# Attention inside a fused attention and two-layer kernel on one Trainium2 core: values as stationary operand on four quarters of the array, weights normalised before the turn, a first stage in three sets of banks and six buffers

## The reference, cut to what matters

```python
# batch 4, heads 8, sequence 768, head_dim 64, 8 memory keys; chunks of 32 queries
for c in range(24):
    q_c    = q[:, :, 32*c : 32*c+32]
    k_full = concat(mem_k, k[:, :, max(0, 32*c-16) : min(768, 32*c+40)])   # up to 64 keys
    v_full = concat(mem_v, v[the same rows])
    scores = q_c @ k_full.T / 8
    a = exp(scores - max(scores));  a = a / (sum(a) + 1e-9)
    out[chunk c] = a @ v_full
x = out as 3072 tokens x 512
x = (sigmoid(x @ w_gate) * (x @ w_val)) @ w_out          # d_ff 1536
h = x @ w_in                                             # d_ff 2048
return (P(h) / (Q(h) + 1e-6)) @ w_out2                   # P cubic, Q quadratic
```

## Time and profile before

| | |
|---|---|
| time before, median of 3 | 1200.07 us (1199.81 to 1202.33) |
| the profiled execution, its own time | 1198.92 us |
| its span, first to last instruction | 1196.6 us, mean granted clock 0.998 |
| PE busy | 1168.5 us, 98% |
| PEld, DVE, ACT, POOL busy | 957.1, 904.0, 751.8, 120.7 us |
| stage 0's units, up to the first product of the first chain | 0 to 61.89 us |
| the two stretches of units between chains | 207.48 to 269.89 and 419.70 to 482.19 us |

### The profile page before, as it was taken

How to read it: one execution, slowest core, us unless ns; L and a number is a source line. 1 busy time by engine, 2 the same in 40 slices (tenths; PEclk the granted TensorE clock), 3 DMA queues, 4 the chain that set the end, 5 groups by cost and what they waited for, 6 DMA issues and landing times.

```text
span 1196.6 us, 21070 instructions
## 1 busy us (share of the span) xinstructions
PE 1168.5 (98%) x8160; PEld 957.1 (80%) x8160; DVE 904.0 (76%) x1387; ACT 751.8 (63%) x1224; POOL 120.7 (10%) x150
## 2 busy tenths in 40 slices
PE   8899999899999998999999999999999999999998
PEld 7778888677888866788887888888888888888887
DVE  3686566567666655776558899998998998988987
ACT  2465555455555544555556787877877877877875
POOL 2122322002322200232300000000000000000000
PEclk9999999999999999999999999999999999999999
DMA  8411411742241174332208300200200200200000
GB/s 281 156 53 65 156 54 53 259 144 79 98 168 53 54 256 137 106 132 81 88 18 290 132 1 1 71 1 1 71 0 0 70 0 0 70 0 0 36 1 35
DMA packets 40720, 97.79 MB, mean 82 GB/s; under 512 B 4288, under 2 KB 4288, under 8 KB 40640
## 3 DMA queue, kind: packets, MB, share of 16 engines
q1 hardware_dynamic: 40640, 96.68, 23.6%
HBM read 84.09 MB, written 12.58 MB: 81 GB/s over the span
## 4 chain that ended last, share of the span: by engine, by line
PE 57%; DVE 1%; DMA 1%; SPq 0%; issue 0%; ACT 0%; ACTq 0%
PE ps_h L1263 7%; PE ps_h L1258 7%; PE ps_h L1259 7%; PE ps_y L1302 7%; PE ps_y L1298 7%; PE ps_y L1296 7%; PE ps_h L1152 3%; PE ps_h L1159 3%; PE ps_h L1154 3%; PE ps_y L1197 1%; PE ps_y L1202 1%; PE ps_y L1198 1%; DMA oraw<-wo_l 1%; PE ps_y L1188 0%; PE ps_y L1292 0%; PE ps_y L1290 0%
## 5 line engine op out<-in xcount | busy, mean ns | idle before, releaser
L1152 PE MATMUL ps_h<-xop,wop 128*128 128x512 f32 x504 | 197.2, 391 | 2.9 <-DVE x_raw L809 2.6
L1154 PE MATMUL ps_h<-xop,wop 128*128 128x512 f32 x504 | 196.2, 389 | 0.0
L1159 PE MATMUL ps_h<-xop,wop 128*128 128x512 f32 x504 | 155.9, 390 | 0.0
L1258 PE MATMUL ps_h<-x_split,weights 128*128 128x512 f32 x384 | 149.4, 389 | 0.0
L1259 PE MATMUL ps_h<-x_split,weights 128*128 128x512 f32 x384 | 149.4, 389 | 0.0
L1296 PE MATMUL ps_y<-weights,hid 128*128 128x512 f32 x360 | 140.0, 389 | 0.0
L1298 PE MATMUL ps_y<-weights,hid 128*128 128x512 f32 x360 | 140.0, 389 | 0.0
L788 DVE TENSOR_TENSOR wop<-rawp,wop 128x448 fp32r<-128x448 f32 x144 | 90.9, 660 | 56.6 <-ACT wop L441 56.5
L809 DVE TENSOR_TENSOR x_raw<-ps_h,probs_t 128x512 f32<-128x512 f32 x72 | 49.5, 688 | 87.0 <-PE ps_h L1159 86.6
L675 ACT ACTIVATE tmp<-ps_h 128x512 f32<-128x512 f32 x96 | 57.2, 595 | 92.4 <-PE ps_h L1263 92.4
L1152 PEld LDWEIGHTS ps_h<-xop,wop 128*128 128x128 f32 x504 | 94.6, 188 | 25.3 <-DVE x_raw L809 4.3
(11 more groups left out here) (89 smaller groups left out, 2254.4 us busy)
## 6 DMA issues: line engine op xcount, KB each, us to landing
rawp<-wgv_l SPq DMA_DIRECT2D x36, 512.0 KB, 3.5
oraw<-wo_l SPq DMA_DIRECT2D x72, 256.0 KB, 3.7
unit<-v_l SPq DMA_DIRECT2D x24, 520.0 KB, 5.8
unit<-k_l SPq DMA_DIRECT2D x24, 512.0 KB, 5.7
unit<-q_l SPq DMA_DIRECT2D x24, 256.0 KB, 4.4
x_stage<-y_dram SPq DMA_DIRECT2D x6, 1024.0 KB, 6.0
out<-stage SPq DMA_DIRECT2D x24, 256.0 KB, 2.2
braw<-wb_l SPq DMA_DIRECT2D x11, 512.0 KB, 5.5
```

The source lines that it names most:

```text
L1152: nc.tensor.matmul(dst, w_h[k], xop[:, m, 0, k, :], start=first and k == 0, stop=False, skip_group_check=True)
L1154: nc.tensor.matmul(dst, w_l[k], xop[:, m, 0, k, :], start=False, stop=False, skip_group_check=True)
L1159: last = nc.tensor.matmul(dst, w_h[k], xop[:, m, 1, k, :], start=False, stop=k == 1, skip_group_check=True)
L1258: nc.tensor.matmul(dst, lhs(c, 0), x_split[:, 0, c, :], start=(c == 0), stop=False)
```

## The change

What it does, on each engine:

- The weights are normalised on DVE right after the exponential (a row sum by `tensor_reduce` takes the place of the column of ones, then + 1e-9, reciprocal, multiply), in the units at the sequence's ends after a `memset` of the keys that do not exist. Then they are turned once.
- `weigh_values` has the values stationary (64 x 64) and the turned weights moving (32 columns); row group and bank alternate with the chunk, so that four 64 x 64 quarters are used. Its output is already turned: `stage_x` reads it, and the second `turn` is gone. The scores' products alternate the two banks with the chunk too. The host orders chunks and keys to suit and leaves the column of ones out (512 instead of 520 KB of values to a unit).
- Stage 0: three sets of banks (the third in `ps_y`), six load buffers, loads queued in one go (q and k of unit 6 wait for scores 0, v of unit 6 for the values' products of unit 0), loop written out without fills; warm-up products: 9 ahead, none later. The first chain stands directly behind the last unit's values.
- Stages 1 and 2: still two sets and two buffers; new order of units and thirds, all 36 thirds inside the stretch (4 behind the last values); the splits of `w_out` and the loads are placed anew; the load of the sigmoid table moves from `last_operands` to behind `split_x(T4, 1)` in the first `quad_a` of a stage; in the very first one two pieces of value weights are split there as well.

```diff
+SETS, BUFFERS = 3, 6
+        ps_att = [ps_h[:, 0:2, 0:256], ps_h[:, 2:4, 0:256], ps_y[:, 0:2, 0:256]]
+        def set_of(g):
+            return (g + 1) % SETS if g < UNITS else g % 2
 SP:
+            load_qk(0)
+            load_qk(1)
+            load_v(0)
+            for g in range(2, UNITS):
                 load_qk(g)
+                load_v(g - 1)
+                if g == 4:
+                    load_raw(0)
+            load_v(UNITS - 1)
+            load_raw(1)
 ACT, stage 0:
+            for g in range(UNITS):
+                if g >= 2:
+                    stage_x(g - 2)
+                if g >= 1:
+                    copy_turned(g - 1)
+                exp_scores(g)
+                if g >= 4:
+                    split_w(0, g - 4)
+                if g == 6:
+                    split_x(0, B11)
+            stage_x(UNITS - 2)
+            copy_turned(UNITS - 1)
+            split_x(0, B21)
+            split_x(0, T2, 0)
+            split_x(0, T1, 0)
+            split_x(0, B22, 0)
+            stage_x(UNITS - 1)
 DVE:
             def normalize(g):
+                b, tile = set_of(g), g // B
+                pr = probs[b].rearrange("p h s k -> p s h k")
+                dve.wait_ge(exped, g + 1)
+                if tile == 0:
+                    nc.vector.memset(probs[b][0:CHUNK, :, :, NMEM:NMEM + LEFT], 0.0)...
+                elif tile == NT - 1:
+                    nc.vector.memset(probs[b][P - CHUNK:P, :, :, KEYS - RIGHT:KEYS], 0.0)...
+                nc.vector.tensor_reduce(row[b], pr, AX.X, ALU.add)...
+                nc.vector.tensor_scalar(row[b], row[b], 1e-9, None, ALU.add)...
                 nc.vector.reciprocal(row[b], row[b])...
+                nc.vector.tensor_tensor(pr, pr, row[b] (broadcast), ALU.mult).then_inc(norm_done, 1)
 DVE, stage 0:
+            for g in range(UNITS):
+                if g:
+                    normalize(g - 1)
+                softmax(g)
+                if g >= 5:
+                    split_w(0, g - 5)
+            split_x(0, B11)
+            normalize(UNITS - 1)
+            split_w(0, 3)
+            split_x(0, B21)
+            token_sum(0, T1, 0)
+            token_sum(0, T2, 0)
 DVE and ACT, last_operands(0): split_w(1, 0) and split_w(1, 1) inside; quad_a(0): split_w(1, 2), split_w(1, 3)
 PE:
             def weigh_values(g):
                 for h in range(HP):
                     for c in range(CT):
                         for e in range(2):
+                            rows = slice(KEYS * ((e + c) % 2), KEYS * ((e + c) % 2 + 1))
+                            cols = slice(D * h + CHUNK * (c // 2), D * h + CHUNK * (c // 2 + 1))
+                            last = nc.tensor.matmul(ps_att[b][D * e:D * (e + 1), c % 2, cols],
+                                                    v_sb[at][rows, c, h, :],
+                                                    probs_t[b][rows, h, CHUNK * c:CHUNK * (c + 1)], ...)
 PE, stage 0:
-            warm_up(2 * WARM)
-            attention(0, lambda: warm_up(WARM))
-            warm_up(4 * WARM)
+            warm_up(3 * WARM)
+            for g in range(UNITS):
+                scores(g)
+                if g >= 2:
+                    weigh_values(g - 2)
+                if g >= 1:
+                    turn(g - 1)
+            weigh_values(UNITS - 2)
+            turn(UNITS - 1)
+            weigh_values(UNITS - 1)
+            chain(0, -1)
 PE, stages 1 and 2, for each pair a, b:
                     scores(a)
+                    if p:
+                        turn(b - 2)
+                    fill()
+                    fill()
                     if p:
+                        weigh_values(b - 2)
                     fill()
+                    fill()
                     scores(b)
+                    turn(a)
                     fill()
                     fill()
                     weigh_values(a)
                     fill()
+                    if p < UNITS // 2 - 1:
+                        fill()
+                turn(first + UNITS - 1)
+                fill()
+                weigh_values(first + UNITS - 1)
+                for _ in range(4):
+                    fill()
...
```

More of the change, by code:

```diff
@@ L319, in _ @@
                 n, g = piece_of(s, 0, TA - 2), UNITS * (s + 1)
+                load_oraw(n + 4)
                 load_qk(g + 2)
-                for ahead in (4, 5, 6):
-                    load_oraw(n + ahead)
+                load_oraw(n + 5)
+                load_oraw(n + 6)
                 load_qk(g + 3)
@@ L401, in exp_scores @@
             def exp_scores(g):
-                b = g % 2
+                b = set_of(g)
                 act.wait_ge(shifted, g + 1)
@@ L505, in quad_a @@
                     split_x(s, T4, 1)
+                    nc.scalar.preload_act_table_set("sigmoid_and_others")
+                    if u == 0:
+                        split_w(cv, 2)
                     snapshot(cg, 2)
+                    if u == 0:
+                        split_w(cv, 3)
                     split_wout(n + 2)
@@ L889, in attention @@
                     a, b = first + 2 * p, first + 2 * p + 1
-                    if p:
-                        normalize(b - 2)
                     softmax(a)
                     at(p, 0)
-                    softmax(b)
                     normalize(a)
                     at(p, 1)
-                normalize(first + UNITS - 1)
+                    softmax(b)
+                    at(p, 2)
+                    normalize(b)
             def last_operands(s, between):
@@ L1119, in warm_up, with chain @@
                 for _ in range(products):
-                    nc.tensor.matmul(ps_y[:, 0, 0:P], ident[:], ident[:], start=True, stop=True)
-            def chain(c, n):
+                    nc.tensor.matmul(ps_y[:, 3, 0:P], ident[:], ident[:], start=True, stop=True)
+            def chain(c, n, places=range(PROD)):
                 u, kind = divmod(c, 2)
@@ L1126, in chain @@
                 pe.wait_ge(w_lo, 4 * (c + 1))
-                for m, (w, name, first) in enumerate(STEPS):
+                for m in places:
+                    w, name, first = STEPS[m]
                     if m == M1:
@@ L1238, in _ @@
                     u, n = NQ * s + i, first_piece(s, i)
-                    chain(2 * u, n)
+                    if u:
+                        chain(2 * u, n)
                     chain(2 * u + 1, n + 1)
```

284 lines of the change are left out of this document (134 added, 150 removed).

## The result

The changed kernel takes 1193.83 us (median of 11 runs, 1191.26 to 1198.72), the kernel before 1201.09 on the same chip (11 runs, 1199.81 to 1203.38): ratio 0.9937, 95% interval 0.9924 to 0.9951.

What follows compares the result with a forecast made beforehand. PE, busy 98% of the span, bounds the kernel; stage 0 is bound by a unit's round through PE, DVE and ACT. Gains 7.0 (stage 0) + 3.2 (PE work) + 4.6 (waits) = 14.8 give 1185.3 us; range 1174 to 1197.

Steps and rivals of the forecast that it cites:

- Stage 0, the rounds: Stage 0, units: the DVE, ACT, DVE round limits, 4.1 us per unit with memset and 3.9 without; last normalize ends at 39.1.
- Stage 0, the loss: Stage 0: instruction-fetch stops of PE and its low clock together cost 3.3 us, bounds 0 and 10; stage 0 gains 7.0.
- Rival (a): Stage 0 starves or runs at low clock: loss 10 us instead of 3.3, time 1192 us; chance 0.17.
- Stage 0, the first chain: From last normalize to M4 of the first chain: 22.3 us, behind DVE's queue; M4 at 61.4, gain 10.3 us before losses.
- Middle stretches, PE work: Middle stretches: a turn goes, the values' new form costs 0.2 us more; net -0.2 us per unit, 16 units, 3.2 us.
- rival (b): Values' products at 20 ns each: 0.45 us more per unit for 16 units, time 1192.5 us; chance 0.10.
- rival (c): Scores and values: row groups writing one bank take turns, 1.8 us more per unit, 29 in all, time 1215 us; chance 0.08.
- Middle stretches, waits: Middle stretches: PE waits 2.3 us less per stretch, 4.6 us in all, bounds 0 and 7.
- Edits at nothing: M6's operand after the last values, table load, load order, host layout: hidden or free, 0 us.
- up to 2 us a stage without cover: Chains behind the middle stretches: possible loss if PE's work does not cover the wait for M6's operand, up to 2 us.

Runs made afterwards that it cites:

- e2: Changed kernel whose stage 0 loads only units 0 and 1 and computes the other six units with their data; ratio to the kernel before 0.9885.
- e14: e11 with two buffers for the units' data and six warm-up products ahead of the first scores instead of nine; median 1184.13 us, ratio 0.9869.
- e1: Changed kernel with warm-up products back in stage 0: 3 before and 4 behind each turn, 6 on either side of the last; ratio 0.9953.
- e5: Changed kernel with two ScalarE passes moved up at stage 0's end: B21's high part and the first weights of chain 1; ratio 0.9921.
- e15: e11 with GpSimd's weight sums put off in stage 0 as well; median 1182.37 us, ratio 0.9854.
- e11: Changed kernel with the edits of e5 and e8 and an earlier ScalarE snapshot of each stage's first M1; median 1183.39 us, ratio 0.9832.
- e8: Changed kernel with GpSimd's weight sums for the second pair of chains of stages 1 and 2 put after the first chain's second sum; ratio 0.9906.
- e12: e2 with the warm-up products of e1 added in stage 0; ratio 0.9899.
- e4: Kernel before, without the warm-up products between the units of stage 0; ratio 1.0008.

## Why the prediction was wrong, step by step

*Stage 0, the rounds: right as a mechanism.* 4.1 and 3.9 us came out as 4.12 and 3.88 once the queue was empty (e2), and as 3.87 in the kernel after from 38.6 us on.

*Stage 0, the loss: the step that failed.* The prediction had the last normalize end at 39.1 and M4 start at 61.4 without any loss, and took 3.3 for stops and clock together, out of bounds of 0 and 10: 2.8 for the clock (eight times 0.35), which leaves half a microsecond for all stops. Measured: the normalize ends at 47.19, 8.1 later, and M4 starts at 71.53, 10.1 later. 6.3 of it are stops under the load queue (e2 against the kernel after). 1.8 is what e2 still has: its last normalize ends at 40.87, not 39.1; the first starts 0.8 late (not surely for the nine warm-up products: with six the first scores waited for their data, e14), and the rest is the low clock of the first rounds. The prediction named the stop of 2.61 us, took it rightly for a fetch of instructions behind data, and then weighed it as a single event in 10 us of full queue; the chance of one per unit was kept as a bound. What the row should have suggested is a rate: PE's instructions come in packets for 127 products. Before, one such place (222) lay under the full queue; after, four (221, 348, 476, 603), of 0.3, 1.7, 2.0 and 1.9 us. Stops and clock were also added as independent terms; under the full queue they are not, since there the packets set the round at either clock (e1). Rival (a), 1192 at 0.17, is what happened, but its loss of 10 was 8.1 of stops and clock and 2.0 of something else:

*Stage 0, the first chain: right in its shape, 2.0 us short.* From the last normalize to M4 it is 24.3 us in the kernel after and in e2, against a forecast of 22.3. VectorE's queue releases M4, as said, and the four products from M6 on cost nothing at half clock. Both long waits of DVE were in the forecast: 2.25 us for a pass of ScalarE (B21) that was queued behind the copy of the last turn, and 2.69 for the weights, which let DVE go on 8.4 us after the normalize instead of 7.7. The other 1.3 are in the 22 operations behind (15.2 us for 13.9), with waits of 0.69, 0.78 and 0.32 for ScalarE. What the prediction didn't ask is whether the two long waits had to be: the data of B21 were ready long before, and e5 took 3.6 us of the way. With these waits gone GpSimd's sums were on the path, 2.2 us (e15 against e11).

*Middle stretches, PE work: right.* 56.75 to 55.19 and 56.83 to 55.67 busy: 1.6 and 1.2 us, forecast 1.6 each. The values' form, timeline of PE in the first middle stretch:

```profile
216.03 1.14 PE L1171 MATMUL ps_h<-probs_t,unit 64*64 64x32 f32 x64
217.09 0.50 PE L1256 MATMUL ps_y<-hid,wout 128*128 128x512 f32 x1
...
219.14 0.86 PE L1147 MATMUL ps_h<-unit 64*32 64x64 f32 x64
219.93 0.66 PE L1157 MATMUL ps_h<-ident,probs 128*128 128x128 f32 x4
```

1.06 us to the next instruction instead of 0.79, 0.27 more where 0.2 was taken and 0.65 was rival (b)'s. The scores, now with two row groups in one bank, are 0.79 to the next as before. So rival (c) is out; and the sentence of the Trainium skill (TensorEngine Tiling (Array Packing), Gotcha 1: PSUM Pressure) that speaks for it doesn't hold for tiles on separate partitions of a bank, as far as time tells.

*Middle stretches, waits: 6.3 instead of 4.6.* Idle time of PE fell from 5.66 to 2.42 and from 5.66 to 2.58 us. What is left in the first is stops in the scores and two turns:

```profile
PE ps_h L1147 <- issue: 1.4, 2, 0.9
PE ps_h L1157 <- DVE probs L797: 1.1, 2, 0.7
```

*Edits at nothing: 4.5 us lost.* The prediction asked whether the operand of M6 and the table load were hidden, and let the load queue's new order pass with one sentence on the units' own q and k. The raw weights behind them, and GpSimd, which starts as soon as they land, had no sentence. e8 and e11 show that this was it, with the snapshot's place as the second part. The "up to 2 us a stage without cover" is the right size (2.5 and 2.0), with another cause.

In sum: 14.8 forecast; stage 0 gave 6.9 less, the middle 1.3 more, the chains 4.5 less; 4.7 by this sum, 4.8 in the traces, 7.3 between the medians (single executions of the kernel after range over 7 us; turn 8 of the same stage 0 stood at 47.25, 47.73, 47.92 and 48.35 in four traces, chiefly because the first stop, ahead of product 221, took 0.3 us in one and about 1 in the others).

## What to carry to other kernels

A stop of PE for nothing that the profile shows, while a load queue is full, is a rate and not an event: count PE's products between the stops, look for the packets of the instruction queue, and price each further block (here 127 products: 6.0 to 6.3 us under the full queue, 4.0 to 4.9 without) before loads are queued in one go or products are added that nobody uses. When a change lets a transfer land earlier, follow who starts on it, up to the engine that shares a port with the critical one. And before PE is blamed for a chain, read the queue of the engine that feeds it for passes whose data are ready and whose place is late.

## What the hardware showed that was not expected

- PE's instructions have a price of their own: small products in large numbers use up a packet of 16 KB per 127, and stops of up to 1.49 us come even with no load under way (e12).
- Warm-up products in a round that PE nearly fills cost more (3.1 us over eight units, e12 against e2, in the two rounds with such stops) than the low clock that they cure (1.3).
- The granted clock isn't always seen: in e4, where a turn takes 1.12 us and the window's clock says 1.00, the instructions' durations are the safer reading. The window and a turn:

```profile
10.00:44.00 34.00, 22.89 (x736) 17.37 (x720) 14.15 (x29) 10.49 (x19) 5.64 (x8) 1.00 0.74 244
...
29.19 1.12 PE L1100 MATMUL ps_h<-ident,probs 128*128 128x128 f32 x4
```

- GpSimd's passes of 256 columns take 0.74 us alone and 1.06 to 1.19 beside VectorE, so that putting them off made them faster too: eight of them in 6 us in e8, and 7.5 in the kernel before.
